# Attention and two MLP layers in one Trainium2 kernel: token sums from half the operands, the inverse root by Newton steps on VectorE, and GpSimd's two small steps exchanged

## What is computed

```python
def _attn_ref(q, k, v):                      # q, k, v: 4 x 8 x 576 x 64
    scores = scale * np.matmul(q, k.transpose(0, 1, 3, 2))
    mask = (rel >= 0) & (rel < window)       # window = 64
    scores = np.where(mask, scores, -1000000000.0)
    scores = scores - np.max(scores, axis=-1, keepdims=True)
    attn = np.exp(scores)
    attn = attn / (np.sum(attn, axis=-1, keepdims=True) + 1e-09)
    return np.matmul(attn, v)

def _moe_ref(x, w_gate, w_val, w_out, rms_g):   # x: 2304 tokens x 512
    rms = np.sqrt(np.mean(x * x, axis=-1, keepdims=True) + 1e-06)
    xn = x / rms * rms_g
    g = xn @ w_gate                              # 512 x 1536
    silu = g * (1.0 / (1.0 + np.exp(-g)))
    return silu * (xn @ w_val) @ w_out           # 1536 x 512

def _moe2_ref(x, w_in, w_out):                   # 512 x 2048, 2048 x 512
    r = np.maximum(x @ w_in, 0.0)
    return r * r @ w_out
```

## Time and profile before

| | |
|---|---|
| median of three runs | 874.08 us (872.70 to 874.89) |
| profiled execution, its own time | 876.73 us |
| its span, first to last instruction | 875.0 us |
| PE busy | 855.9 us (98%) |
| DVE, ACT, POOL busy | 589.8, 478.3, 471.8 us |
| PE's granted clock, mean | 0.99 |

### The profile page before, as it was taken

How to read it: one execution, slowest core, us unless ns; L and a number is a source line. 1 busy time by engine, 2 the same in 40 slices (tenths; PEclk the granted TensorE clock), 3 DMA queues, 4 the chain that set the end, 5 groups by cost and what they waited for, 6 DMA issues and landing times.

```text
span 875.0 us, 16811 instructions
## 1 busy us (share of the span) xinstructions
PE 855.9 (98%) x6388; PEld 843.9 (96%) x6388; DVE 589.8 (67%) x729; ACT 478.3 (55%) x1005; POOL 471.8 (54%) x473
## 2 busy tenths in 40 slices
PE   6898999999999999999999999999999999999998
PEld 5687999999999999999999999999999999999998
DVE  3758766558658547755547867678577777577972
ACT  5777665644566645455555455554555454555451
POOL 3656488674489756378867368322177212386100
PEclk8989999999999999999999999999999999999999
DMA  8863122211322122222222322257622266522587
GB/s 284 255 208 105 43 73 73 66 50 61 90 73 72 57 61 61 73 73 73 73 73 61 81 63 75 61 157 222 223 74 74 76 204 198 171 73 97 180 263 231
DMA packets 108015, 100.18 MB, mean 114 GB/s; under 512 B 6944, under 2 KB 85920, under 8 KB 107936
## 3 DMA queue, kind: packets, MB, share of 16 engines
q1 hardware_dynamic: 92544, 84.04, 32.2%
q10 hardware_dynamic: 15392, 15.08, 5.0%
HBM read 79.69 MB, written 19.40 MB: 113 GB/s over the span
## 4 chain that ended last, share of the span: by engine, by line
PE 93%; DVE 3%; ACT 1%; issue 1%; DMA 1%; POOL 0%; DVEq 0%; POOLq 0%; ACTq 0%
PE banks L848 29%; PE banks L849 29%; PE banks L850 29%; PE banks L807 2%; ACT probs L1163 1%; DVE probsT L1495 1%; PE banks L749 1%; PE banks L781 1%; PE banks L821 1%; DMA w_kept<-stash 1%; DVE acts L1435 0%; DVE banks L1475 0%; PE banks L757 0%; DVE xc_lo L1626 0%; DVE h L1603 0%
## 5 line engine op out<-in xcount | busy, mean ns | idle before, releaser
L848 PE MATMUL banks<-xc_hi,w_hi 128*128 128x384 f32 x844 | 282.7, 335 | 0.2 <-DVE xc_lo L1467 0.2
L850 PE MATMUL banks<-xc_hi,w_lo 128*128 128x384 f32 x844 | 281.9, 334 | 0.0
L849 PE MATMUL banks<-xc_lo,w_hi 128*128 128x384 f32 x844 | 281.9, 334 | 0.0
L848 PE MATMUL banks<-hs_hi,d_hi 128*128 128x384 f32 x544 | 182.2, 335 | 0.1
L850 PE MATMUL banks<-hs_hi,d_lo 128*128 128x384 f32 x544 | 181.7, 334 | 0.0
L849 PE MATMUL banks<-hs_lo,d_hi 128*128 128x384 f32 x544 | 181.7, 334 | 0.0
L848 PEld LDWEIGHTS banks<-xc_hi,w_hi 128*128 128x128 f32 x844 | 158.4, 188 | 0.6 <-DVE xc_lo L1467 0.4
L849 PEld LDWEIGHTS banks<-xc_lo,w_hi 128*128 128x128 f32 x844 | 158.4, 188 | 0.0
L850 PEld LDWEIGHTS banks<-xc_hi,w_lo 128*128 128x128 f32 x844 | 158.4, 188 | 0.0
L1412 DVE TENSOR_TENSOR w_lo<-w_raw,w_hi 128x1024 fp32r<-128x1024 f32 x58 | 77.1, 1330 | 82.3 <-ACT w_hi L1094 82.2
L574 POOL TENSOR_TENSOR w_raw<-w_raw 128x256 f32<-128x256 f32 x58 | 62.7, 1081 | 120.5 <-DVE d_lo L1581 52.2
(11 more groups left out here) (114 smaller groups left out, 1349.6 us busy)
## 6 DMA issues: line engine op xcount, KB each, us to landing
w_kept<-stash SPq DMA_DIRECT2D x56, 256.0 KB, 3.2
w_raw<-in_w_gate SPq DMA_DIRECT2D x36, 256.0 KB, 2.9
w_raw<-in_w_val SPq DMA_DIRECT2D x72, 128.0 KB, 2.8
d_raw<-in_w_out SPq DMA_DIRECT2D x36, 256.0 KB, 2.7
d_raw<-in_w_down SPq DMA_DIRECT2D x32, 256.0 KB, 2.8
v_sb<-in_v_rows SPq DMA_DIRECT2D x16, 384.0 KB, 4.9
w_raw<-in_w_in SPq DMA_DIRECT2D x24, 256.0 KB, 2.7
w_raw<-in_w_in SPq DMA_DIRECT2D x48, 128.0 KB, 2.6
```

What stands on the lines that cost most here:

```text
L848: pe.matmul(ps, w_h, v_h, start=first, stop=False, skip_group_check=joined)
L849: pe.matmul(ps, w_h, v_l, start=False, stop=False, skip_group_check=joined)
L850: return pe.matmul(ps, w_l, v_h, start=False, stop=last, skip_group_check=joined)
```

## The change

1. `ones` is the first constant POOL writes, with a semaphore of its own (`ones_set`). PE's warm-up multiplies `ones` by `ones`, nine times, and starts on that semaphore; four such matmuls more follow the scores of slot 0, six more those of slot 1 (`FILL`).
2. POOL's two small steps change places in every slot: first the maximum of group g is scaled, then 1e-9 is added to the sums of group g-1.
3. Squares are made two rows of channels at a time in one instruction. The squares of channels 0 to 255 and 256 to 511 are then added (POOL in slot 10 for the first 384 tokens, DVE in slot 12 for the others), so that `first_sums` takes two matmuls for each 128 tokens instead of four. It takes them against 64 columns of `ones` instead of one, and stands in slots 11 and 13 instead of 10 and 12.
4. ACT's square root and DVE's reciprocal go. `inverse_root` on DVE makes the inverse root with seven small instructions, each waiting for the one before: a first guess from the bits, and two Newton steps. This holds for the two later pairs too, within the runs.
5. The diagonals of the first pair are made in two halves, in slots 13 and 14.
6. The rounding of step 1's weights on POOL goes from slot 10 to 12, the remainders from slots 14 and 15 to 15 and 16.

The diff, cut to what the text speaks of:

```diff
-WARM = 6
+WARM = 9
+FILL = {0: 4, 1: 6}
+WIDE = 64
+ROOT_SEED = float(0x5F1FFFF9)
+ROOT_STEPS = ((-0.703952253, 0.703952253 * 2.38924456), (-0.5, 1.5))
+STEPS = 1 + 3 * len(ROOT_STEPS)
...
         def _(pool):
+            nc.gpsimd.memset(ones[:], 1.0).then_inc(ones_set, 1)
...
-            pool.wait_ge(consts, step)
-            nc.gpsimd.memset(ones[:], 1.0).then_inc(consts, 1)
...
+            def first_diagonals(c):
+
+                n = TB // 2
+                pool.wait_ge(rinv_done, STEPS)
+                pool.wait_ge(ms_mm, 1)
+                nc.gpsimd.tensor_tensor(diag[0][:, c * NT:(c + 1) * NT].rearrange("p (n c) -> p n c", n=n),
+                                        ident[:].unsqueeze(1).broadcast_to([P, n, P]),
+                                        guess[:, c * n:(c + 1) * n].unsqueeze(2).broadcast_to([P, n, P]),
+                                        ALU.mult).then_inc(diag_done, 1)
...
-            def square_half(k, c):
-                of = half_cols(0, k, c)
-                nc.gpsimd.tensor_tensor(squares[0][k][:, c * NT:(c + 1) * NT], of, of, ALU.mult).then_inc(sq_pool, 1)
+            def square_two(kh, c):
+                of = x_block(0, kh, c)
+                nc.gpsimd.tensor_tensor(sq_all[:, 2 * kh:2 * kh + 2, c * NT:(c + 1) * NT], of, of,
+                                        ALU.mult).then_inc(sq_pool, 1)
 
             for g in range(TAIL):
                 n = g - N_LAG
-                if 0 <= n < GROUPS:
-                    total = sums[:, n % PR, :]
-                    pool.wait_ge(exp_done, n + 1)
-                    nc.gpsimd.tensor_scalar(total, total, 1e-9, None, ALU.add).then_inc(summed, 1)
                 if g < GROUPS:
                     peak = neg_max[:, g % PR, :]
                     pool.wait_ge(maxed, g + 1)
                     nc.gpsimd.tensor_scalar(peak, peak, SCALE, None, ALU.mult).then_inc(biased, 1)
                 if 0 <= n < GROUPS:
+                    total = sums[:, n % PR, :]
+                    pool.wait_ge(exp_done, n + 1)
+                    nc.gpsimd.tensor_scalar(total, total, 1e-9, None, ALU.add).then_inc(summed, 1)
                     pool.wait_ge(inverted, n + 1)
...
                 if g in (8, 9):
                     pool.wait_ge(o_out, O_DONE[A_GROUP + 1])
-                    for k in (2 * (g - 8), 2 * (g - 8) + 1):
-                        square_half(k, 0)
+                    square_two(g - 8, 0)
                 if g == 10:
+                    pool.wait_ge(sq_pool, 2)
+                    nc.gpsimd.tensor_tensor(sq_all[:, 0:2, 0:NT], sq_all[:, 0:2, 0:NT], sq_all[:, 2:4, 0:NT],
+                                            ALU.add).then_inc(sq_added, 1)
+                if g == 11:
+                    pool.wait_ge(o_out, O_DONE[B_GROUP + 1])
+                    square_two(0, 1)
+                if g == 12:
                     high1_plain(1)
                     high2_plain(1)
...
             def slot(g):
                 if g < GROUPS:
                     if g == 0:
+                        pe.wait_ge(ones_set, 1)
+                        for n in range(WARM):
+                            pe.matmul(bank[5][:, 0:P], ones[:], ones[:], start=True, stop=True)
                         pe.wait_ge(consts, 6)
-                        for n in range(WARM):
-                            pe.matmul(bank[5][:, 0:P], ident[:], ident[:], start=True, stop=True)
...
-                    for k in range(KT):
-                        mm = pe.matmul(ps[:, n:n + 1], squares[0][k][:, n * P:(n + 1) * P], ones[:, 0:1],
-                                       start=k == 0, stop=k == KT - 1)
+                    for k in range(2):
+                        mm = pe.matmul(ps[:, n * WIDE:(n + 1) * WIDE], squares[0][k][:, n * P:(n + 1) * P], ones[:, 0:WIDE],
+                                       start=k == 0, stop=k == 1)
...
                 slot(g)
-                if g == 10:
+                for n in range(FILL.get(g, 0)):
+                    pe.matmul(bank[5][:, 0:P], ones[:], ones[:], start=True, stop=True)
+                if g == 11:
                     pe.wait_ge(consts, CONSTS)
-                    pe.wait_ge(sq_pool, KT)
+                    pe.wait_ge(sq_added, 1)
                     first_sums(0, bank[5])
-                if g == 12:
-                    pe.wait_ge(sq_pool, KT + 2)
-                    pe.wait_ge(sq_done, 2)
+                if g == 13:
+                    pe.wait_ge(sq_added, 2)
                     first_sums(1, bank[5])
...
-                if g == 12:
-                    root(0)
...
+            def inverse_root(q):
+
+                done = STEPS * q
+                dve.wait_ge(ms_done, q + 1)
+                nc.vector.tensor_scalar(guess[:].bitcast(I32), rms[:].bitcast(I32), -0.5, ROOT_SEED, ALU.mult,
+                                        ALU.add).then_inc(rinv_done, 1)
+                for n, (by, plus) in enumerate(ROOT_STEPS):
+                    dve.wait_ge(rinv_done, done + 1 + 3 * n)
+                    nc.vector.tensor_tensor(resid[:], guess[:], guess[:], ALU.mult).then_inc(rinv_done, 1)
+                    dve.wait_ge(rinv_done, done + 2 + 3 * n)
+                    nc.vector.scalar_tensor_tensor(out=resid[:], in0=resid[:], scalar=by, in1=rms[:], op0=ALU.mult,
+                                                   op1=ALU.mult).then_inc(rinv_done, 1)
+                    dve.wait_ge(rinv_done, done + 3 + 3 * n)
+                    nc.vector.scalar_tensor_tensor(out=guess[:], in0=resid[:], scalar=plus, in1=guess[:], op0=ALU.add,
+                                                   op1=ALU.mult).then_inc(rinv_done, 1)
...
                 if g == 12:
+                    dve.wait_ge(sq_pool, 3)
+                    dve.wait_ge(sq_done, 1)
+                    nc.vector.tensor_tensor(sq_all[:, 0:2, NT:PW], sq_all[:, 0:2, NT:PW], sq_all[:, 2:4, NT:PW],
+                                            ALU.add).then_inc(sq_added, 1)
+                if g == 13:
                     mean_square(0, bank[5])
-                if g == 13:
-                    inverse(0)
+                    inverse_root(0)
```

More of the change, by code:

```diff
@@ L30 @@
 BF16 = mybir.dt.bfloat16
+I32 = mybir.dt.int32
 ALU = mybir.AluOpType
@@ L205, in build @@
         rms = sb("rms", [P, TB], F32)
+        guess = sb("guess", [P, TB], F32)
+        resid = sb("resid", [P, TB], F32)
         assert top[0] <= nc.sbuf_usable_end, (top[0], nc.sbuf_usable_end)
         T1, T2, T3, T4 = [sb(f"T{n + 1}", [P, PW], F32, temp_at + n * PW * 4) for n in range(4)]
-        squares = [[sb(f"sq{n}_{k}", [P, PW], F32, at + k * PW * 4) for k in range(KT)]
-                   for n, at in enumerate((hs_at, h_at + C1 * PW * 4))]
+        sq_all = sb("sq_all", [P, KT, PW], F32, hs_at)
+        squares = [[sq_all[:, k, :] for k in range(KT)],
+                   [sb(f"sq{k}", [P, PW], F32, h_at + (C1 + k) * PW * 4) for k in range(KT)]]
         diag = [sq[0] for sq in squares]
@@ L1111, in high2 @@
                 copy(w_hi[u % 2][:, G1:G1 + G2], w_raw[u % 2][:, HALF_K + G1:HALF_K + G1 + G2], hi2_done)
-            def square_half(k, c):
-                cols = slice(c * NT, (c + 1) * NT)
-                nc.scalar.activation(squares[0][k][:, cols], half_cols(0, k, c), ACT.Square).then_inc(sq_done, 1)
             def square(q, k):
                 nc.scalar.activation(squares[1][k][:], pair_cols(q, k), ACT.Square).then_inc(sq_done, 1)
-            def root(q):
-                act.wait_ge(ms_done, q + 1)
-                nc.scalar.activation(rms[:], rms[:], ACT.Sqrt).then_inc(rms_done, 1)
             def gate_plain(u, c):
@@ L1168, in _ @@
                     act.wait_ge(o_out, O_DONE[B_GROUP + 1])
-                    square_half(2, 1)
-                    square_half(3, 1)
-                if g == 12:
-                    root(0)
+                    nc.scalar.activation(sq_all[:, 2:4, NT:PW], x_block(0, 1, 1), ACT.Square).then_inc(sq_done, 1)
                 if g in (15, 16):
```

39 lines of the change are left out of this document (17 added, 22 removed).

## The result

| | before | after |
|---|---|---|
| median of 16 runs each | 874.70 us (872.70 to 877.33) | 876.23 us (875.20 to 880.31) |
| ratio, 95% interval | | 1.0028 (1.0017 to 1.0039) |
| profiled execution: own time, span | 876.73, 875.0 us | 879.01, 877.3 us |
| PE, DVE, ACT, POOL busy | 855.9, 589.8, 478.3, 471.8 us | 853.2, 598.6, 470.7, 474.3 us |

The kernel became slower by 0.28% (0.17 to 0.39%), some 2.4 us by this ratio, while the two medians differ by 1.5 us. The sum had made it 2 us faster. The median lies inside the range, 4.1 us above the 872.1. The profiled execution of after lies 2.8 us above its median, that of before 2.0 us above its own.

What follows compares the result with a forecast made beforehand. PE bounds the products after 86 us; before, no engine is full and DVE sets the pace from 66 us. -1.0 - 1.85 + 0.2 + 0.68 = -1.97 us: 876.73 becomes 874.8, median 872.1, range 868.0 to 876.5 us.

Steps and rivals of the forecast that it cites:

- Within the runs: Products after the slots: DVE's small instructions, about 1.6 us in each of two steps, are covered: 0, bounds 0 to +3.2.
- from slot 17 to the 64 outputs: Slot 17 to the first products: one more POOL step on the sums lies in DVE's way, +0.68 us.
- Up to slot 8: Early slots: warm-up +0.4, POOL's new order -1.3, filling matmuls up to -1 us; -1.9 halved to -1.0, between +0.8 and -3.0.
- The halving for the stops: Before slot 8: PE's stops without a semaphore swallow half of the 1.9 us gain, leaving -1.0.
- Slots 9 to 11: Two slots of DVE's loop at 3.35 us and slot 11 at 4.45 make 11.15 instead of 13.0 us: -1.85.
- Slots 12 to 17: DVE's own work at base 3.28 us a slot sums to 23.4 us, before 23.2: +0.2.
- The exchange: POOL's swapped small steps: inversion 1.29 us after the maximum's start instead of 0.61, 0.68 longer; 1.3 us gained in slots 1 and 2.
- The exchange costs little: Rival, chance 0.25: if ACT sets the late slots, six times 0.68, 4.1 us, fall away: 868.0 us.
- The exchange costs in every slot: Rival, chance 0.14: DVE is the bound from slot 4 on, 14 times 0.68 = 9.5 us: 876.9 us.
- The clock falls all the same: Rival, chance 0.11: 64 columns are too few, half-clock stretches stay, about 0.9 us each: 873.9 us.
- DVE and POOL collide: Inside the likeliest case (0.50): the new sum of squares may take the longer time, +0.5, 872.6 us.
- The signs: Right: no half clock behind sums, inversion at 1.3 us, first product near 80.3; uncovered: PE idle over 5 us after 86 us.

Runs made afterwards that it cites:

- newton_after_step: Changed kernel with the later pairs' Newton steps placed on DVE behind the step that makes `va`, one step earlier: 874.44 us, ratio 1.0002.
- changed_again: The changed kernel run unaltered once more, for a second profiled execution: 877.16 us, ratio 1.0022.
- scale_first_to_slot_2: Changed kernel with POOL's scale first only in slots 0 to 2, and the later Newton steps moved behind `va`: 869.64 us, ratio 0.9943.
- act_root_in_runs: Changed kernel with ACT's square root and DVE's reciprocal back for the two later pairs, Newton kept for the first: 873.81 us, ratio 0.9998.
- sum_first: Changed kernel with POOL's two small steps back in their old order, the step on the sums before the scale: 874.16 us, ratio 0.9993.

## Why the prediction was wrong

**Within the runs: the step that failed.** "The products in work cover both: 0" is 2.5 us (787.4 against 784.9). PE's two waits for `va` are 1.9 of it; its weight loads, which wait for the same `va`, show the 2.5. Two runs that only take the Newton steps out of `va`'s way gain 0.26% and 0.30%. It lay in the step's own bounds (0 to 3.2 us), but my value was the wrong end. The new work on DVE was priced at 1.6 us a step. DVE's timeline of after:

```profile
157.64 0.98 DVE L1445 TENSOR_SCALAR guess<-rms 128x6 int32<-128x6 int32 x1
158.66 0.65 DVE L1449 TENSOR_TENSOR resid<-guess 128x6 f32<-128x6 f32 x1
159.35 0.17 DVE L1451 SCALAR_TENSOR_TENSOR resid<-resid,rms 128x6 f32<-128x6 f32 x1
159.55 0.59 DVE L1454 SCALAR_TENSOR_TENSOR guess<-resid,guess 128x6 f32<-128x6 f32 x1
...
161.59 0.55 DVE L1692 TENSOR_TENSOR va<-banks,c_u 128x384 f32<-128x384 f32 x1
```

The same of before:

```profile
157.04 0.18 DVE L1432 RECIPROCAL rms<-rms 128x6 f32<-128x6 f32 x1
157.55 0.56 DVE L1657 TENSOR_TENSOR ga<-banks,c_t 128x384 f32<-128x384 f32 x1 [0.32 <-PE banks L850]
158.59 0.56 DVE L1665 TENSOR_TENSOR va<-banks,c_u 128x384 f32<-128x384 f32 x1 [0.48 <-PE banks L850]
```

POOL of after at that time:

```profile
156.92 1.68 POOL L708 TENSOR_TENSOR h<-sbb,vb 128x384 f32<-128x384 f32 x1 [0.89 <-ACT sbb L1216]
158.56 0.73 POOL L587 TENSOR_TENSOR w_raw<-w_raw 128x256 f32<-128x256 f32 x1
159.37 0.75 POOL L591 TENSOR_TENSOR w_raw<-w_raw 128x256 f32<-128x256 f32 x1
```

Four of the seven instructions take 0.59 to 0.98 us instead of 0.17, and each long one ends within 0.03 us of the end of a POOL instruction (158.62 and 158.60, 159.31 and 159.29, 160.14 and 160.12). Together they take 3.5 us, not 1.6. Measured from `w_lo` ahead of it, which began 0.60 us later in after, `va` is 3.0 - 0.6 = 2.4 us late; PE waited 0.95, so the cover was some 1.5 us. Seven steps in 1.4 us, with the wait of 0.32 ahead of `ga` used up first, would have stayed inside it; this is reckoned, not run. That they grow by waiting for POOL is read from the ends of the rows, and from the same instructions while POOL was idle: 0.17 us for the five in newton_after_step, and 0.17 us for all seven in slot 13 of after, where POOL did nothing from 59.10 to 62.34 us. No run took away POOL's work in step 9 itself. The Trainium skill, page "SBUF — State Buffer", section "Who interferes with whom", says that a DVE instruction with two SBUF inputs and a GpSimd instruction that reads SBUF exclude each other; the three long steps of two inputs agree. The fourth, the guess from the bits, has one input and waited longest; no sentence that I cite covers it. I had weighed the rule for the sum of squares alone, and not for instructions of six elements, where the wait is two and a half to five times the work.

**The slots: the rest of the miss.** By the medians (1.5 us in all, 2.5 of it within the runs) the slots gained 1.0 us, by the ratio (2.4 in all) 0.1, where I had 1.97. So even with the 2.5 us in their place my sum would have come to +0.5 us, no change, and not to what was measured. The marks of the sum, from DVE's merges (their starts in slots 9, 12 and 17) to the 64 outputs:

| | forecast | after | changed_again |
|---|---|---|---|
| up to the merge of slot 9 (41.35 before) | -1.0 | 38.84: -2.5 | 38.77: -2.6 |
| slots 9 to 11 (13.0) | -1.85 | 11.73: -1.3 | 11.48: -1.5 |
| slots 12 to 17 (23.2) | +0.2 | 26.80: +3.6 | 23.26: +0.1 |
| from slot 17 to the 64 outputs (11.73) | +0.68 | 12.52: +0.8 | 13.87: +2.1 |
| sum | -1.97 | +0.6 | -1.9 |
| behind the 64 outputs (785.7) | 0 | 787.4: +1.7 | 788.9: +3.2 |

Of the 3.2 us in the last row 1.3 are one wait for a DMA. That the slots of changed_again come to my sum is luck: -2.6 and +2.1 stand where I had -1.0 and +0.68.
- *Up to slot 8*: of its parts, the 1.3 us of the exchange in slots 1 and 2 do not show in the traces (scale_first_to_slot_2). The filling matmuls, "worth up to 1 us", come out at 2.0 to 2.5 in the changed kernel and at 1.2 in the one before, both with wide intervals. The halving for the stops was too careful.
- *Slots 9 to 11*: the quiet loop was 3.37 to 3.61 for my 3.35, the 12 passes 1.52 for 1.4.
- *Slots 12 to 17*: the terms of DVE are right where nothing stops PE (23.3 also in act_root_in_runs). The 26.8 of after hold stops of 0.90 and 2.10 us and half a clock. I had read stops only where before had them, ahead of slot 8, and gave them no bound behind it. The mean and the seven small instructions take 1.6 us, 0.20 apart, for my 1.95 (by my own rule of 0.10 on top of 0.16 I should have had 0.26 each and not 0.24). The sum of squares is 1.36 us in after for my 0.95, and 0.95 in changed_again, where POOL's rounding of weights beside it took 1.56 instead of 0.82: one or the other was the longer.
- *The exchange*, 0.68 us a slot: 0.76 at the inversion, and 0.79 from merge to merge (4.43 instead of 3.64 us in slots with two normalisations, newton_after_step and sum_first). In the table's row from slot 17 on, 0.79 stands for the 0.68 and, in changed_again, 1.35 us more for the half clock behind the longer wait. This last I had in no term; it stands in five of eight executions. Counted as 4.7 us less half of 1.3, it was 4.0; the runs give 3.1 and 3.3.

**The rivals.** *The exchange costs little* fell: the inversion is 1.37 us behind the maximum in every late slot. *The exchange costs in every slot*, with 876.9 us, has the number (876.2) but not the mechanism: 3.1 us, not 9.5. *The clock falls all the same* had a wrong condition. The clock went with the number of passes and not with the columns, and the first sums never lost it with 12 of them. What it had in its favour, that PE waits more late in the slots, came true at another place, behind the wait of 2.5 us. *DVE and POOL collide* was right, in the place where I did not look for it.

**The signs.** The inversion came as said, and no half clock stood behind the first sums. It stood behind the second ones in after. PE's first product behind its last wait came at 82.80 us, not near 80.3, and under the 84 of the second rival. PE's idle time behind 86 us was 4.99 us, just under the 5 that I had set as the sign of an uncovered chain, and yet the chain was not covered: the sign was set too high.

**The base.** I carried the profiled execution's surplus over its median to after. The surplus is luck of stops and clock in one execution; the part behind the mark alone repeats.

## What to carry to other kernels

Before new small instructions go on an engine, look at what POOL runs beside it at that moment, and at who waits for the next result: seven instructions of 0.17 us cost 3.5 us on their engine and delayed the result by 2.4; put behind that result instead of ahead of it, they cost nothing. An exchange that shortens a wait where the engines are idle lengthens the loop where they are not; price both stretches apart. Here the lengthening is shown, by 0.35 and 0.38% of the time; that the early slots gain anything by the exchange is not. When a change carries several edits, find a mark in the trace behind which the time repeats from run to run, and compare the two parts separately.

## What the runs showed of the hardware

- PE stops without a semaphore ahead of the same seven instructions in ten executions of one instruction order, for 0 to 2.5 us, differently in each execution, all before 60 us; none was seen in the 785 us of products. In the stops of 0.9 us and more the DMA engines are 0.7 busy or more, but ahead of the 9 or 10 scores, in six stops of 0.17 to 0.82 us, they do next to nothing (0.00 to 0.07). So a load on the DMA engines is no condition for a stop. I take the stops for instruction fetch, which is argued from their fixed places and not shown. The Trainium skill, page "Runtime: NRT & Kernel Launch", section "Instruction fetch mechanics", calls its cost mostly hidden: if they are fetches, here it isn't, with up to 6.7 us of stops in one execution.
- Seven small instructions on DVE, 128x6, take 0.17 us each while POOL is idle, and four of them 0.59 to 0.98 us beside POOL's instructions, each ending with one of these.
- Behind a single wait of 2.5 us, with no work on PE, PE had half its clock for 3.4 us (6.8 in one) in five of eight executions, which made the products 0.32 us apart instead of 0.17 and cost 1.35 us (from the outputs ahead to the mark: 10.35 us in changed_again, 9.00 in after); behind one of some 1.65 us in none of six.
- Whether 12 passes have 1 or 64 columns, they take 0.12 us each, and the clock behind them was alike. Behind 24 in a row it was half in eight cases of eight, behind 12 in two of twenty.
